# Issuing the later batches' loads one at a time on the sync queue

## The reference

```python
def _attn_ref(q, k, v, alpha):            # (4, 8, 768, 48) each
    for t in range(S):
        state = alpha[:, :, t, :, None] * state + einsum('bhd,bhe->bhde', k[:, :, t], v[:, :, t])
        y[:, :, t] = einsum('bhd,bhde->bhe', q[:, :, t], state)

def _moe_ref(x, U, V, w_ch1, w_ch2):      # x (4, 768, 384), rank 32, hidden 1536
    u = x + ((x.transpose(0, 2, 1) @ U) @ V).transpose(0, 2, 1)
    return u + np.maximum(u @ w_ch1, 0.0) @ w_ch2

def _moe2_ref(x, w_in, w_spatial, b_spatial, w_out):
    h = np.maximum(x @ w_in, 0.0)          # 1024 wide, halves u and v
    v_n = layer_norm(v); v_s = w_spatial @ v_n + b_spatial
    return (u * v_s) @ w_out
```

## Time and profile before

| | us |
|---|---|
| median of 3 runs (761.78 to 770.37) | 766.34 |
| the profiled execution | 764.89 |
| its span, first to last instruction | 763.1 |
| PE busy | 717.8 |
| DVE, ACT, POOL busy | 349.4, 330.8, 201.6 |

### The profile page before, as it was taken

The page is one execution under the profiler, slowest core; times in us unless marked ns, Lnnn a source line. Parts: engine busy times, 40 slices in busy tenths (PEclk is TensorE's granted clock), DMA queues, the critical chain, the costliest instruction groups (busy, mean ns, idle before and its releaser), DMA issues.

```text
span 763.1 us, 25662 instructions
## 1 busy us (share of the span) xinstructions
PE 717.8 (94%) x11408; PEld 678.8 (89%) x11408; DVE 349.4 (46%) x607; ACT 330.8 (43%) x576; POOL 201.6 (26%) x141
## 2 busy tenths in 40 slices
PE   1678899999999989999999999999999999999998
PEld 1577789899898879999999899999998998999998
DVE  5997565554655535555463322225314322531531
ACT  4786546436446426446434332226233332322412
POOL 5511372130251210063130233331240140033021
PEclk9999999999999999999999999999999999999999
DMA  9415601301401221301000232212012002001001
GB/s 282 147 28 180 166 3 39 120 22 39 137 3 39 74 65 39 111 30 39 4 34 2 74 125 63 73 44 113 1 42 84 1 22 103 0 0 62 0 0 62
DMA packets 15692, 47.12 MB, mean 62 GB/s; under 512 B 1680, under 2 KB 8080, under 8 KB 15088
## 3 DMA queue, kind: packets, MB, share of 16 engines
q1 hardware_dynamic: 15600, 45.73, 19.0%
HBM read 36.29 MB, written 9.44 MB: 60 GB/s over the span
## 4 chain that ended last, share of the span: by engine, by line
PE 88%; DVE 3%; ACT 2%; issue 2%; DVEq 0%; ACTq 0%
PE HB L807 26%; PE ZB L807 9%; PE ZB L884 7%; PE ZB L886 7%; PE ZB L885 7%; PE SB L807 6%; PE SB L684 4%; PE ZB L920 3%; PE HB L920 3%; PE SB L789 2%; PE SB L920 2%; PE SB L798 2%; PE HB L925 2%; PE ZB L925 2%; PE SB L744 1%
## 5 line engine op out<-in xcount | busy, mean ns | idle before, releaser
L1394 DVE SCALAR_TENSOR_TENSOR hid_lo<-HB,hid_hi 128x384 fp32r<-128x384 f32 x96 | 53.3, 556 | 153.4 <-ACT hid_hi L1112 152.6
L1112 ACT ACTIVATE hid_hi<-HB 128x384 fp32r<-128x384 f32 x96 | 47.4, 493 | 165.0 <-PE HB L807 164.8
L807 PE MATMUL HB<-uh,w1h 128*128 128x384 f32 x288 | 104.2, 362 | 7.4 <-issue 4.7
L884 PE MATMUL ZB<-hid_hi,w2h 128*128 128x384 f32 x288 | 98.9, 343 | 1.0 <-issue 1.0
L807 PE MATMUL HB<-ul,w1h 128*128 128x384 f32 x288 | 98.0, 340 | 0.0
L807 PE MATMUL HB<-uh,w1l 128*128 128x384 f32 x288 | 97.7, 339 | 0.0
L886 PE MATMUL ZB<-hid_lo,w2h 128*128 128x384 f32 x288 | 96.8, 336 | 0.0
L885 PE MATMUL ZB<-hid_hi,w2l 128*128 128x384 f32 x288 | 96.4, 335 | 0.0
L967 ACT COPY Qd<-Q 48x768 f32<-48x768 f32 x84 | 72.9, 868 | 16.8 <-PE SB L684 8.9
L637 POOL TENSOR_TENSOR gl<-gated,gh 128x384 fp32r<-128x384 f32 x32 | 32.4, 1014 | 179.2 <-ACT gh L1127 179.2
L606 POOL TENSOR_TENSOR Q<-Q,bk 112x768 f32<-112x768 f32 x14 | 26.1, 1868 | 173.3 <-ACT Qd L967 173.3
(11 more groups left out here) (227 smaller groups left out, 1473.8 us busy)
## 6 DMA issues: line engine op xcount, KB each, us to landing
Q<-in_q SPq DMA_DIRECT2D x8, 672.0 KB, 7.6
AL<-in_al SPq DMA_DIRECT2D x7, 672.0 KB, 5.6
K<-in_k SPq DMA_DIRECT2D x7, 672.0 KB, 4.7
Vt<-in_v SPq DMA_DIRECT2D x8, 576.0 KB, 8.5
mid<-x2s SPq DMA_DIRECT2D x8, 576.0 KB, 4.0
x<-mid SPq DMA_DIRECT2D x4, 1152.0 KB, 5.7
out<-o_sb SPq DMA_DIRECT2D x24, 192.0 KB, 1.8
x2s<-in_w SPq DMA_DIRECT2D x9, 384.0 KB, 3.4
```

The costliest lines, as they stand in the source:

```text
L807: last = nc.tensor.matmul(dst, weights(x, w), moving(y, m), start=(n == 0 and x == y == 0), stop=(n == total - 1 and y == 1))
L884: nc.tensor.matmul(bank, w2h[:, i, cols], hi, start=(i == 0), stop=False)
L1112: nc.scalar.activation(hid_hi[:, i % HID, :], HB[i % 2][:, 0:TILE], ACT.Relu).then_inc(h_hi, 1)
L1394: nc.vector.scalar_tensor_tensor(hid_lo[:, i % HID, :], HB[i % 2][:, 0:TILE], 0.0, hid_hi[:, i % HID, :].bitcast(F32), ALU.max, ALU.subtra ...
```

## The change

From group (1, 0) on, SP waits after each load until it has landed before it issues the next. The wait for K's landing stands before whatever follows K in SP's order: the w2 pieces for group (1, 0), a store of the block's result for the others. Before the loads of group (b+2, 0) SP also waits until the first half's store has landed. The loads themselves, their order, and the loads of batch 0 are the same; the parameter `first` of `load_group` is gone. PE, DVE, ACT and POOL have the same instructions in the same order as before.

```diff
-            def load_group(a, g, first):
-                load_decay(a, g, first)
-                load_queries(a, g, first)
+            def load_group(a, g):
+                load_decay(a, g, False)
+                sp.wait_ge(ld_al[g], 16 * (a + 1))
+                load_queries(a, g, False)
+                sp.wait_ge(ld_q[g], 16 * (a + 1))
                 load_values(a, g)
-                load_keys(a, g, first)
+                sp.wait_ge(ld_v[g], 16 * (a + 1))
+                load_keys(a, g, False)
+                sp.wait_ge(ld_k[g], 16 * (a + 1))
...
-            load_group(1, 0, False)
+            load_group(1, 0)
             for n in range(W1_PIECES + STAGE, NW1):
                 load_piece(n)
             for b in range(BATCH - 1):
                 load_queries(b + 1, 1, False)
+                sp.wait_ge(ld_q[1], 16 * (b + 2))
                 load_values(b + 1, 1)
+                sp.wait_ge(ld_v[1], 16 * (b + 2))
                 load_decay(b + 1, 1, False)
+                sp.wait_ge(ld_al[1], 16 * (b + 2))
                 load_keys(b + 1, 1, False)
+                sp.wait_ge(ld_k[1], 16 * (b + 2))
                 store_mid(b, range(0, 1))
                 if b < BATCH - 2:
-                    load_group(b + 2, 0, False)
+                    sp.wait_ge(mid_stored[0], 16 * b + 32)
+                    load_group(b + 2, 0)
                 store_mid(b, range(1, QT))
```

## The result

The changed kernel is faster by about half a per cent: 759.03 us (median of 19 runs, 755.8 to 766.49) against 762.94 us (19 runs, 759.09 to 770.79), ratio 0.9945 with a 95% interval of 0.9923 to 0.9968. That is 4.2 us (0.0055 x 762.94), between 2.4 and 5.9. The spread is narrower as well: the sixteen fastest runs lie within 4.1 us (755.8 to 759.87), where those of before take 7.9 (759.09 to 766.99); the full ranges, with the few long runs, are 10.7 and 11.7 us. The profiled execution took 759.09 us.

A forecast was written before the change was run, and what follows sets the result against it. The prediction took PE to bound the kernel, busy 717.8 of 763.1 us. A 2.9 us price less a 5.96 us gain gave -3.1 us, so the 766.34 us median became 763.3 us, range 759 to 771.

The forecast's parts named there:

- The reading of the stall: PE's 4.74 us idle to 270.40 us: an instruction fetch on q8 stood behind loads SP had stacked on q1.
- The first rival: Stacking does not delay fetches, so only PE's wait for K near 79 us is left: 769.2 us; chance 0.24.
- The price of the first group: Group (1, 0): K lands at 82.9 us, PE waits 3.6 us, 0.7 comes back; net 2.9 us (0.8 to 6.3).
- the 0.7 us of the forecast: Step 1 of group (1, 0): its 0.68 us standstill at 85.39 us would be absorbed once step 0 starts later.
- The clock: Around K's wait: set at nothing; a new 0.50 spell may cost 1.22 us, while step 0's present spell would fall into the wait.
- The other groups: Groups (2, 0) to (3, 1): the waits cost nothing, with 13 us of cover at (2, 0).
- The gain: From 265.66 us on: the long stall, 4.74 us, and its slow matmul unit, 1.22, go; 5.96 us in all.
- three small pieces: PE's issue pieces at L684 beside the other stacks, 1.4 us in sum; left in place, kept as an end of the range.
- the second: Rival: w2 pieces and Q of (1, 1) pile up at 83 us, holding a fetch another 5.96 us: 769.2 or 775 us; chance 0.11.
- the third: Rival: K at its early bound, small pieces gone too, -6.6 us: 759.8 us; a stall-richer median run gains more; chance 0.13.
- One sign of being wrong: In the changed profile: a long PE issue piece beside loads that run alone; no size given.
- The sum: Whole kernel: 2.9 - 5.96 = -3.1 us, median 763.3 us, -0.4%.

The follow-up runs named there:

- stacked copies: Kernel before plus eight 672 KB query copies, issued with no wait behind the Vt loads of four later groups: 1.0234, 779.12 us.
- waits at the later groups: Changed kernel, but group (1, 0)'s four loads go out with no wait, as before: 0.9905, 757.11 us; again on another chip 0.9888, 757.04 us.
- K fourth: Kernels with the changed kernel's order in group (1, 0), AL, Q, Vt, K, each waited for; the changed kernel itself 0.9945, 759.03 us.
- first group alone: Changed kernel with the new waits kept only at group (1, 0)'s four loads, all others taken out: 1.0000, 764.58 us.
- no store wait: Changed kernel without the wait for the store's landing ahead of the loads of (2, 0) and (3, 0): 0.9968, 762.84 us.
- waited copies: Changed kernel plus eight 672 KB query copies behind the Vt loads of four later groups, each waited for: 0.9985, 761.63 us.
- K third: Changed kernel with K ahead of Vt in group (1, 0), each still waited for: 0.9902, 0.9945 and 0.9890 in three runs (756.93, 757.43, 756.77 us).
- parts: Changed kernel, K ahead of Vt in (1, 0), loads from (1, 1) on in halves, stores in thirds, nearly all waited for: 0.9923, 756.30 us.
- both stores waited for: Changed kernel, K ahead of Vt in (1, 0), second half's store also waited for ahead of Q of (2, 1), (3, 1): 0.9941, 761.69 us.

## Why the prediction was right or wrong

Two stretches of SP's timeline separate price and gain in all fourteen profiled executions: from AL of (1, 0) to K of (1, 1), which ends with PE's work on group (1, 0), and from there to the last first-half store of the attention part (381.48 us before). Before, for instance, 119.99 - 63.75 = 56.24 and 381.48 - 119.99 = 261.49.

| kernels (executions) | AL (1, 0) to K (1, 1), us |
|---|---|
| group (1, 0) at once: before, stacked copies, two with waits at the later groups | 56.24, 53.52, 54.52, 53.75: median 54.1 |
| K fourth: the change twice, first group alone, no store wait, waited copies | 55.22, 59.57, 56.56, 58.63, 56.04: median 56.6 |
| K third: three times, parts, both stores waited for | 52.37, 55.43, 54.24, 53.84, 54.73: median 54.2 |

| kernels (executions) | K (1, 1) to the store, us |
|---|---|
| old order of issue: before, first group alone | 261.49, 264.09 |
| the change's waits: the change twice, later groups alone twice, K third three times, waited copies | 255.24, 256.39, 256.87, 254.64, 256.16, 256.16, 254.46, 255.40: median 255.8 |
| no store wait; parts; both stores waited for; stacked copies | 259.28; 261.24; 261.28; 269.48 |

- **The reading of the stall** was right. The 4.74 us were a fetch behind q1's transfers: the run without the store wait, the stacked and the waited copies show it. All sixteen issue pieces of 0.9 us or more between 140 and 335 us in the fourteen executions end 2.3 to 2.8 us after a q8 packet starts; PE's waits for K end 8.7 us or more after the last one. The first rival, that the stack does not matter, falls with the gain and with the two runs of copies. The Trainium skill's rule on turns packet by packet (DMA: Bandwidth & Descriptors, "Queues, rings and completion order") does not agree with the 515 packets of q1 without one of q8, if the profile's packets are those of the rule and the fetch was due before them; the measurement decides. Turns of a coarser kind, a transfer at a time, are not excluded.
- **The price of the first group**, 2.9 us net, was nearly right in size: 56.6 - 54.1 = 2.5 us by the first table. What it is made of was wrong, so the size is partly luck. PE waited 2.6 us where 3.6 was forecast, mostly since Vt landed in 3.6 us and not 4.5 (1.8 to 4.3 us in the five executions with K fourth). But nearly all of this wait comes back, more than the 0.7 us of the forecast. PE's idle time in the stretch, its length less PE's busy time, is 7.4 us by the median with K fourth and 7.2 with the group at once, where three of the four executions lose 1.6 us at step 1 to ACT's Qd. The price lies in busy time, 48.6 against 46.5 us for the same work. The stretch in the changed kernel, and with waits at the later groups alone (busy of PE first, PEclk third from the end):

```profile
65.23:120.45 55.22, 48.37 (x1007) 44.38 (x1004) 33.31 (x44) 30.24 (x54) 29.48 (x18) 0.94 0.38 115
64.06:118.58 54.52, 46.39 (x988) 42.39 (x989) 33.88 (x44) 30.38 (x54) 28.73 (x18) 1.00 0.40 116
```

- **The clock**, which the prediction set at nothing, is thus most of the price. It expected the slow spell of step 0 to fall into the wait; step 0 took 1.51 us after the change as before, against 1.03 for step 1. All five executions with K fourth have a stretch at 0.50, the 1.2 GHz level, around the wait (mean granted clock 0.86 to 0.97); the nine others have it there in three. What brings it on is not shown. In the two executions that the result shows, the price is hidden (55.22 against 56.24) by chance: the kernel before ran at 0.50 a second time, from 109.34 to 112.75 us; its 1.0 us at L884 is missing from the three other executions with the group at once too; and the wait at L741, 0.6 against 1.5 us (a piece that the prediction's list of PE's waits left out), was 1.5 in the second profile of the change.
- **The other groups** cost nothing, as forecast: no wait of PE after 90 us names a load or ends with one's landing.
- **The gain** was 5.96 us in the forecast, read from one execution. By the second table it is 262.8 - 255.8 = 7.0 us (262.8 is the mean of the two old-order executions, 2.6 us apart, so this is rough), and that is where most of the difference lies. For the execution that was read it is 261.5 - 255.8 = 5.7. It is idle time of PE, 6.7 and 7.6 us against 1.1 to 2.9, and a stretch at 0.50 behind each long stall, which the eight executions with the change's waits do not have. Of the three small pieces that the prediction left in place, the first, near 150 us, stands in all fourteen executions with 0.6 us, 4.4 to 5.3 us after a fetch starts, so it is no such stall. Of the two others, 0.4 us each, one is gone in both profiles of the change, and the other is 0.2 and 0.4 us there. The sum, 2.5 - 7.0 = -4.5, agrees with the 4.2 us measured; forecast was -3.1.
- **The rivals**: the pile of pieces and Q at 83 us made no stall (no piece over 0.25 us between 84 and 109 us in the changed kernel's two profiles), so the second falls. Of the third, K at an early bound and more stalls in a usual run, a part came true. One sign of being wrong, a long issue piece beside loads that run alone, is there in the 1.4 us of the change's second profile and with both stores waited for.
- **The step that failed** is the sum of price and gain, and what was made of it. The mechanism held, but the gain was put too low (5.96 us, measured 7.0) and the price too high (2.9, measured 2.5), so -3.1 us stand against the 4.2 us that were measured. And from three runs that spread over 8.6 us the prediction took 1% as the limit of what can be told, so it filed a gain of 0.4% under no change that can be told, at 0.80. Nineteen runs of each tell 0.23% either way, and the gain of 0.55% is clear of that. The spread was no fixed noise of the measurement: part of it, it seems, were the stalls that the change removes, as the prediction's own third rival said, since most runs lie closer together after it. The absolute range, 759 to 771, held the median by 0.03 us only, since it hung on a median of three that stood 3.4 us above that of nineteen.
- **Too narrow** was the word "stack". One transfer in flight when the fetch falls due can hold it up too; a stack makes the hold longer and surer. That would explain why the parts and the second store wait, each of which takes away a stack or shortens a transfer, gave nothing or lost; it is argued, not shown.

## What to carry to other kernels

Where PE runs long unrolled code, look for "issue" pieces beside bursts of loads, and set the packets of the instruction queue against those of the loads in the same window: a transfer that nobody waits for can still stop PE. Count the matmuls up to each fetch in several executions: the one that starts late was held up. Spread such loads over the time in which nobody needs them, but keep the one load with little slack (here K of group (1, 0)) ahead in the chain or out of it. Where stalls depend on how transfers fall against fetches, one profile shows one draw; compare stretches over several executions and time many runs.

## What the runs showed of the hardware

An instruction packet on q8 started only as q1's load packets ended, in the run without the store wait (none among 515, then one as 13 small ones were left) and in the run with both stores waited for. It does not wait for a whole stack, though. In the kernel before, the one that ended the long stall started at 267.57 us with 1.09 MB of q1's still to move (DMA, 267.5 to 274 us):

```profile
q1 hardware_dynamic: 247, 1.09, 65.9%
q8 instruction: 2, 0.03, 2.2%
```

And it can start in the midst of a transfer, as at 198.65 us in the changed kernel, among 90 packets of q1 from 198 to 199.5 us. PE's next matmul came 2.3 to 2.8 us after the start of the packet in all sixteen stalls of 0.9 us or more. The store alone, with no load beside it, cost 1.4 us. The price of depth was large: eight copies of 672 KB cost 17.9 us stacked and about 3 to 5 us one by one. And a wait that should only have helped went with a median 5 us higher, by moving three loads 2.6 to 4.7 us later.
